# Two of five row tiles per batch copied out of PSUM by VectorE instead of ScalarE, in the attention stage of an attention, MoE and mixer kernel

## The reference

```python
# 1. attention: a coarse one on means of four tokens, and a banded local one; both summed
out_up = np.repeat(sm_attn(q_d, k_d, v_d), 4, axis=2)          # *_d: means over four tokens
out_local = softmax(where(|i - j| < 4, scale * q @ k.T, -1e9)) @ v
x = (out_up + out_local)  # -> (B, S, H * D)
# 2. mixture of eight experts, one expert a token, chosen by x @ w_gate (or kept from the token before)
out[b, s] = p[e] * (np.maximum(x[b, s] @ w1[e], 0.0) @ w2[e])
# 3. mixer: over tokens, then over channels
u = x + (np.maximum(xt @ w_tok1, 0.0) @ w_tok2).transpose(0, 2, 1)
return u + np.maximum(u @ w_ch1, 0.0) @ w_ch2
```

## Time and profile before

| | us |
|---|---|
| median of three runs | 876.59 |
| lowest and highest | 871.86, 878.53 |
| the profiled execution, its own time | 870.81 |
| its span from first to last instruction | 868.8 |

### The profile page before, as it was taken

The page is one execution under the profiler, slowest core; times in us unless marked ns, Lnnn a source line. Parts: engine busy times, 40 slices in busy tenths (PEclk is TensorE's granted clock), DMA queues, the critical chain, the costliest instruction groups (busy, mean ns, idle before and its releaser), DMA issues.

```text
span 868.8 us, 14419 instructions
## 1 busy us (share of the span) xinstructions
PE 836.5 (96%) x5097; PEld 687.3 (79%) x5098; DVE 393.8 (45%) x789; ACT 333.5 (38%) x855; POOL 214.8 (25%) x320
## 2 busy tenths in 40 slices
PE   8999898987999999999999989999999999999998
PEld 4667676654787888888788868999999889999997
DVE  4877787857543624365643385121123341121211
ACT  4677777652353525355633452111112211111110
POOL 6788888734221122112212100000000000000000
PEclk9999999998999999999999999999999999999999
DMA  9779898410637523455552360011020200010101
GB/s 168 135 127 218 173 212 182 147 55 25 229 117 243 188 90 106 172 186 194 178 167 73 124 215 1 1 34 40 0 73 1 73 1 1 0 37 1 37 1 37
DMA packets 94051, 88.24 MB, mean 102 GB/s; under 512 B 63197, under 2 KB 68975, under 8 KB 93999
## 3 DMA queue, kind: packets, MB, share of 16 engines
q1 hardware_dynamic: 87835, 74.62, 31.7%
q0 software_dynamic: 3760, 12.32, 4.4%
q10 hardware_dynamic: 2404, 0.60, 0.4%
HBM read 72.05 MB, written 15.48 MB: 101 GB/s over the span
## 4 chain that ended last, share of the span: by engine, by line
PE 77%; POOL 5%; DVE 5%; DMA 5%; issue 3%; ACT 3%; SPq 0%; ACTq 0%; POOLq 0%; DVEq 0%
PE scores L1739 11%; PE scores L1740 11%; PE scores L1741 11%; PE bank L1741 6%; PE bank L1739 6%; PE bank L1740 6%; PE bank L1796 4%; PE bank L1803 4%; PE bank L1797 4%; POOL asb L771 2%; DMA stage<-in_moe_w 2%; ACT asb L949 1%; PE scores L1603 1%; PE scores L1787 1%; PE bank L1747 1%
## 5 line engine op out<-in xcount | busy, mean ns | idle before, releaser
L1447 DVE SCALAR_TENSOR_TENSOR h2l<-scores,h2h 128x384 fp32r<-128x384 f32 x72 | 40.1, 557 | 191.9 <-ACT h2h L1097 191.9
L1097 ACT ACTIVATE h2h<-scores 128x384 fp32r<-128x384 f32 x72 | 35.4, 492 | 229.5 <-PE scores L1741 229.5
L1739 PE MATMUL scores<-uTh,W 128*128 128x384 f32 x288 | 98.1, 341 | 0.0
L1740 PE MATMUL scores<-uTl,W 128*128 128x384 f32 x288 | 97.4, 338 | 0.0
L1741 PE MATMUL scores<-uTh,W 128*128 128x384 f32 x288 | 97.0, 337 | 0.0
L1741 PE MATMUL bank<-W,h2l 128*128 128x512 f32 x216 | 84.4, 391 | 0.0
L1739 PE MATMUL bank<-W,h2h 128*128 128x512 f32 x216 | 84.3, 390 | 0.0
L1740 PE MATMUL bank<-W,h2h 128*128 128x512 f32 x216 | 84.1, 389 | 0.0
L1371 DVE TENSOR_TENSOR W<-stage,W 128x1024 fp32r<-128x1024 f32 x56 | 66.7, 1220 | 22.8 <-ACT W L1020 22.3
L1796 PE MATMUL bank<-W,hTh 128*128 128x512 f32 x184 | 76.2, 414 | 0.0
L1020 ACT ACTIVATE W<-stage 128x1024 fp32r<-128x1024 f32 x56 | 57.9, 1055 | 47.0 <-DVE ysb L1396 24.3
(11 more groups left out here) (246 smaller groups left out, 1630.7 us busy)
## 6 DMA issues: line engine op xcount, KB each, us to landing
stage<-in_moe_w SPq DMA_DIRECT2D x56, 512.0 KB, 4.6
vl<-in_v SPq DMA_DIRECT2D x40, 128.0 KB, 3.6
qraw<-in_q SPq DMA_DIRECT2D x32, 144.0 KB, 5.6
v<-in_v SPq DMA_DIRECT2D x8, 576.0 KB
ub<-y_dr SPq DMA_DIRECT2D x18, 256.0 KB, 4.0
out<-ob SPq DMA_DIRECT2D x18, 256.0 KB, 2.1
x_dr<-xrow SPq DMA_DIRECT2D x16, 256.0 KB, 3.5
raw<-in_moe_w SPq DMA_DIRECT2D x8, 512.0 KB, 5.0
```

What stands on the lines that cost most here:

```text
L1097: act.activation(dst, bank[bk][:, 0:width], ACT.Relu).then_inc(relu_hi, 1)
L1447: dve.scalar_tensor_tensor(dst, bank[bk][:, 0:width], 0.0, hi.bitcast(F32), ALU.max, ALU.subtract).then_inc(bank_free, 1)
L1739: pe.matmul(ps, ah, bh, start=first, stop=False)
L1740: pe.matmul(ps, ah, bl, start=False, stop=False)
```

## The change

VectorE gets its own `copy_rows`, with the same wait for a filled bank and for the earlier store of `xrow`, and the same semaphore at its end. It takes the tiles m = 1 and m = 3 of the batches 0, 1 and 2: six copies of 128x512 fp32 from PSUM to SBUF. ACT copies them one step later in its program (step `g`+1, ahead of the exponentials); DVE does it at the end of its own step `g`, behind the k copy and ahead of the weight split. ACT keeps m = 0, 2 and 4, and all of the last batch.

```diff
+def rows_on_vector(b, m):
+
+    return b < B - 1 and m in (1, 3)
...
-                    elif kind == "rows":
+                    elif kind == "rows" and not rows_on_vector(a, i):
                         copy_rows(a, i)
...
+            def copy_rows(b, m):
+                what = ("rows", b, m)
+                dve.wait_ge(side_full, SIDE_AT[what] + 1)
+                if b:
+                    dve.wait_ge(x_out[m], 16 * b)
+                dve.tensor_copy(xrow[0:XM[m], m, :], side_bank(what)[0:XM[m], :]).then_inc(side_sem(what), 1)
+
...
                 for kind, a, i in side_work(g):
                     if kind == "turn" and on_vector(a, i):
                         copy_k(a, i)
+                    elif kind == "rows" and rows_on_vector(a, i):
+                        copy_rows(a, i)
                 for c in split_work(g - 1):
                     split_lo(c)
```

## The result

| | before | change |
|---|---|---|
| median, 20 runs each | 874.33 | 879.17 |
| lowest and highest | 871.47, 878.78 | 874.92, 884.57 |
| profiled execution, its own time (span) | 870.81 (868.8) | 881.12 (879.2) |
| its mean granted TensorE clock | 0.996 | 0.986 |

The ratio is 1.0056 [1.0038, 1.0074]: 4.9 us slower. The prediction had 877.5 with 870.5 to 884 and "within 1%", and its working had 2.3 us of loss. The side is right; the size is half of what came. The profiled execution of the change is a long one: it lies 10.3 us above its counterpart, where the medians lie 4.8 apart. Read it for mechanisms, the medians for sizes.

A forecast was written before the change was run, and what follows sets the result against it. DVE's maxima were taken to bound the affected places; removal 0 and added copies 0.60 + 0.40 + 0.60 + 0.40 + 0.33 + 0 = 2.3 us gave 877.5, a value between 876.5 and 878.9; range 870.5 to 884.

The forecast's parts named there:

- What bounds it: Half batches 2, 4, 6: behind the copies leaving ACT, ACT waits for DVE's maxima (0.76 and 0.29 us idle); DVE ends last.
- the removal: Taking six row copies off ACT in half batches 2, 4 and 6: worth 0, at most 2.6 us saved.
- the 0.43: Time in us an ACT row copy was taken to occupy, start to start, read from the chain of waits in half batch 4.
- ACT's relief pays: Rival, chance 0.13: freed 0.43 us counts at all six places and DVE's copies hide; up to 2.6 us less.
- The copy's price: Each added 128x512 DVE copy from PSUM occupies about 0.60 us, between 0.56 and 0.69.
- The places: Delay of DVE's maxima at m = 1 and m = 3 of half batches 2, 4, 6; sum 2.3 us.
- The cover at m = 3 of half batch 2: DVE's 0.76 us idle before the maxima there hides the 0.60 us copy, so it costs 0.
- POOL's entry at m = 3: Half batch 4: the 0.40 us delay enters by POOL, idle 2.10 us until DVE's reciprocal behind the maxima.
- The first matmul of the experts: Sign to look for behind the attention: it comes 2 to 3 us later in the changed kernel.
- Waits costed at 0: New or moved waits, such as for a filled bank, the earlier store, or the PE's next rows piece: cost 0.
- the clock falls: Rival, chance 0.02: added PE idle lowers the granted clock to 1.2 GHz for one stretch, some 12 us more, 891.
- weight splits collide with POOL: Rival, chance 0.07: in half batches 4 and 6 delayed DVE splits meet POOL's stream, 4 x 0.78 = 3.1 us more, 882.0.

The follow-up runs named there:

- e3: The changed kernel with extra matmuls filling the PE's long waits, nothing else changed; 876.82 us median, ratio 1.0059 to the kernel before.
- e1: The changed kernel with only tile m = 1 copied by DVE, m = 3 back on ACT; 879.98 us median, ratio 1.0102 to the kernel before.
- e2: The changed kernel with only tile m = 3 copied by DVE, m = 1 back on ACT; 876.12 us median, ratio 1.0045 to the kernel before.
- e7: The changed kernel with only tile m = 2 copied by DVE, m = 1 and 3 back on ACT; 874.87 us median, ratio 1.0006 to before.
- e5: The changed kernel run again without an edit, with a second profile; 880.64 us median, ratio 1.0074 to the kernel before.
- e9: The kernel before, with ACT's high weight split of units 40 and 58 cut into three instructions to lengthen the PE's wait; 876.38 us, ratio 1.0046.
- e10: The changed kernel with the PE's waits filled by extra matmuls, repeated for more executions; 877.63 us median, ratio 1.0060 to the kernel before.
- e6: The changed kernel with DVE's k copy of the same step moved to ACT in half batches 3, 5 and 7; 874.26 us, ratio 1.0004 to before.

## Why the prediction was right, and where it was not

- **What bounds it.** Right. Both removed copies stood ahead of an ACT that waits for DVE; the removal was worth 0, and ACT's idle grew as foreseen at m = 1 (some 1.94 forecast, 1.76 measured) and at m = 3 (1.1 forecast, 1.00 in e3), with the clock fall on top in the change (1.60). What an ACT copy occupies was misread: the 0.43 is a piece of the chain, and in order of time it is 0.54. At a worth of 0 this alters nothing; the rival's best case would be 3.2 us in place of 2.6. The rival "ACT's relief pays" is out: e1 and e2 are both slower than before, and it is m = 2 (e7) that gives a lead.
- **The copy's price.** 0.60 taken, 0.60 measured from start to start, and 0.667 to 0.677 recorded against the 0.691 of the earlier trace rows.
- **The places.** Forecast 0.33, 0, 0.60, 0.40, 0.60, 0.40; e3 shows 0.25, 0, 0.54, 0.3, 0.54, 0.3. Sum 1.9 for 2.3. The cover at m = 3 of half batch 2 held, with 0.21 us of DVE's idle left (0.16 forecast). POOL's entry at m = 3 is as foreseen in kind, but its idle of 2.10 became 2.93 in e3, where 0.4 more at most was forecast: the delay of m = 1 arrives there too. The first matmul of the experts, forecast 2 to 3 us later, starts 2.5 later in e3 (212.89) and 6.25 in the change.
- **Waits costed at 0.** The step failed here. I followed the delay along the chain, to "the PE's turn waits for the q copy", and stopped. The same delay makes that one wait of the PE longer, 0.94 to 1.21. In the profiled executions of the change and of e5 the granted clock falls 1.4 and 2.0 us behind its end; most of the other executions have a low mean clock, whose place no trace shows. The fall is worth some 3.6 us over the attention of the profiled execution (5.93, against e3's 2.78 less the 0.45 that only e3 has), a step that the sum didn't have.
- **The rival "the clock falls", given 0.02.** Its mechanism is the right one and was costed on the wrong pattern. I compared the 13.96 busy of 16 us with the 2.06 of 5 us in the earlier trace rows and took the fall to be out of reach. It came in a stretch with the PE busy 2.79 of 4 us around one wait, and not in every execution: e1's profiled one has the same waits of 1.21 and keeps the clock. I also priced it as a whole 16 us stretch at double length, 12 us; it is 10.2 us of the lower level and some 3.5 us of time, since at full clock the PE would have waited for part of it.
- **The rival "weight splits collide with POOL", given 0.07.** It happens, at two places and for 0.93, not at four for 3.1. One of the two is in half batch 7, where I did not look, and the other is a meeting that before had one instruction later: a delay that is carried on changes what meets what later.
- **The share of each.** By the trace without a fall in the attention the change costs 2.8: 1.9 of the forecast's own terms and 0.9 of collisions. At equal mean clock the executions of e5 give 2.2. The difference of the medians is 4.9 and 6.5 in the two sets; the remaining 2.1 to 3.7 go with the mean clock, and e9 shows that a longer PE wait alone can bring such a loss. Not settled: how much of it comes from falls in the attention and how much from DMA waits behind it with falls of their own, and why e3 and e10 stay 5 us above before.
- **The range held** because its width came from the spread of the executions, not because the terms were right.

## What to carry to other kernels

Whether an engine has room is read at the place: DVE, busy for 45% of the span, had 0, 0.20, 0.27 and 0.76 us to spare at four places where the copy went or could go, and only the last took it for nothing. Where a delay ends in a wait of the PE, cost the wait twice, once as time and once as a risk to the granted clock behind it, and compare the mean granted clock over many executions rather than one trace. Before a difference between two traces is put down to a change, follow it along the span: here one DMA wait, in a stage that the change doesn't touch, differed by over 2 us between executions. Where a move costs, take something else off the same engine ahead of the same instruction (e6) before undoing it.

## What the runs showed of the hardware

- A wait of the PE that was 0.2 to 0.3 us longer (0.94 to 1.13 or 1.21), in a stretch where the PE is otherwise busy at the full clock, went with a share of executions with a mean clock of 0.988 or less of 6 of 12 (e9, against 1 of 34 of before in its set) and 25 of 32 (the change, against 8 of 90 in all sets). Each such set has a median 4 to 7 us above that of the others of the same kernel (878.2 and 873.8 for before, 882.6 and 876.8 for e5, 879.8 and 873.1 for e9).
- The fall doesn't always come at the same wait: near 110 in the change and e5, at 140 in e2, at neither in e1's profiled execution, whose attention keeps the full clock.
- How long the lower level lasts says little of what it costs: 10.2 us of it in the attention cost the change some 3.6, and 13.7 us in the routing of e3, where before has 6.8, at most 0.3.
- DVE's 128x512 copy from PSUM recorded 0.667 to 0.677 us and occupied 0.60; ACT's recorded 0.66 and occupied 0.54 (106.49 to 107.03 in before).
- The chain's wait for the store of `y_dr` and its load took 8.6 to 11.9 us, and that for expert weights near 260 us 7.3 to 9.2, over the profiled executions whose chain has them.
- Over a DVE subtraction with two SBUF inputs POOL's multiplication took 1.87 us in place of 1.04, and a subtraction that began inside a POOL instruction took 1.30 with 0.75 of that one to go, 0.80 with 0.25.
